# A fused attention and gated-mixer kernel on one core: groups of the mixer one place later among the heads, spatial groups half by half, and the last mixer in another order

## What is computed

```python
h = np.maximum(x @ w_in, 0.0)                       # 512 -> 1024
u, v = h[..., :512], h[..., 512:]
v_n = (v - mu) / np.sqrt(var + 1e-06)               # over the 512 columns
v_s = np.einsum('ts,bsd->btd', w_spatial, v_n) + b_spatial[None, :, None]
y = (u * v_s) @ w_out                               # 512 -> 512
```

## Time and profile before

| | us |
|---|---|
| median of 3 runs | 867.6 (867.1 to 869.02) |
| the profiled execution, its own time | 869.89 |
| its span in the trace | 868.1 |
| TensorE busy | 836.6 (96%) |
| TensorE weight loads busy | 709.4 (82%) |
| VectorE, ScalarE, GpSimd busy | 348.9 (40%), 290.5 (33%), 203.2 (23%) |

### The profile page before, as it was taken

How to read it: one execution, slowest core, us unless ns; L and a number is a source line. 1 busy time by engine, 2 the same in 40 slices (tenths; PEclk the granted TensorE clock), 3 DMA queues, 4 the chain that set the end, 5 groups by cost and what they waited for, 6 DMA issues and landing times.

```text
span 868.1 us, 13430 instructions
## 1 busy us (share of the span) xinstructions
PE 836.6 (96%) x5064; PEld 709.4 (82%) x5064; DVE 348.9 (40%) x774; ACT 290.5 (33%) x784; POOL 203.2 (23%) x289
## 2 busy tenths in 40 slices
PE   7989999999999999998989999999999999999998
PEld 4766787768877688777969999999999999999997
DVE  5876644365443664417464312213222123122111
ACT  5865654355543554424344111111111111111110
POOL 4874646243341442503341000000000000000000
PEclk9999999999999999999989999999999999999999
DMA  6551321221212221016343003003003002001000
GB/s 212 163 174 42 112 81 42 77 86 58 69 43 76 80 65 42 2 54 194 98 147 114 1 1 109 1 0 109 0 0 109 0 0 90 18 0 43 30 1 36
DMA packets 37681, 56.02 MB, mean 65 GB/s; under 512 B 2749, under 2 KB 20157, under 8 KB 37630
## 3 DMA queue, kind: packets, MB, share of 16 engines
q1 hardware_dynamic: 37630, 55.34, 19.5%
HBM read 45.90 MB, written 9.44 MB: 64 GB/s over the span
## 4 chain that ended last, share of the span: by engine, by line
PE 51%; issue 4%; POOL 1%; DVE 1%; ACT 0%; POOLq 0%; ACTq 0%; DVEq 0%
PE psum L1017 17%; PE psum L1016 17%; PE psum L1015 17%; PE psum L1083 1%; POOL rstd L494 0%; POOL unit_raw L536 0%; DVE mix_buf L820 0%; POOL x_r L503 0%; DVE units_r L864 0%; DVE y_res L921 0%; DVE units_r L866 0%; POOL probs L483 0%; DVE mix_buf L810 0%; ACT x_r L616 0%; ACT units_r L682 0%
## 5 line engine op out<-in xcount | busy, mean ns | idle before, releaser
L908 DVE SCALAR_TENSOR_TENSOR h_r<-psum,h_r 128x384 fp32r<-128x384 f32 x96 | 53.5, 557 | 287.0 <-ACT h_r L709 287.0
L709 ACT ACTIVATE h_r<-psum 128x384 fp32r<-128x384 f32 x96 | 47.2, 492 | 340.5 <-PE psum L1017 340.5
L1015 PE MATMUL psum<-xn_r,units_r 128*128 128x384 f32 x384 | 129.6, 337 | 0.0
L1017 PE MATMUL psum<-xn_r,units_r 128*128 128x384 f32 x384 | 129.3, 337 | 0.0
L1016 PE MATMUL psum<-xn_r,units_r 128*128 128x384 f32 x384 | 128.9, 336 | 0.0
L483 POOL TENSOR_SCALAR probs<-probs,row_inv 128x512 f32<-128x512 f32 (+4 forms) x160 | 95.6, 612 | 139.2 <-DVE row_inv L759 139.2
L569 ACT ACTIVATE probs<-psum,neg_max 128x512 f32<-128x512 f32 (+4 forms) x160 | 89.1, 564 | 95.9 <-DVE neg_max L746 95.7
L746 DVE TENSOR_REDUCE neg_max<-psum 128x1 f32<-128x512 f32 (+4 forms) x160 | 77.6, 535 | 92.5 <-PE psum L938 92.3
L1017 PE MATMUL psum<-units_r,h_r 128*128 128x512 f32 x288 | 113.7, 395 | 0.0
L1016 PE MATMUL psum<-units_r,h_r 128*128 128x512 f32 x288 | 113.5, 394 | 0.0
L1015 PE MATMUL psum<-units_r,h_r 128*128 128x512 f32 x288 | 111.9, 389 | 0.0
(11 more groups left out here) (101 smaller groups left out, 1477.5 us busy)
## 6 DMA issues: line engine op xcount, KB each, us to landing
qk_raw<-qk SPq DMA_DIRECT2D x32, 576.0 KB, 4.0
unit_raw<-w_ch SPq DMA_DIRECT2D x32, 256.0 KB, 3.1
y_norm<-y_scratch SPq DMA_DIRECT2D x6, 768.0 KB, 5.8
y_res<-y_scratch SPq DMA_DIRECT2D x6, 768.0 KB, 4.6
out<-y_res SPq DMA_DIRECT2D x18, 256.0 KB, 2.1
v_raw<-vN SPq DMA_DIRECT2D x16, 256.0 KB, 3.0
y_scratch<-mix_buf SPq DMA_DIRECT2D x16, 256.0 KB, 2.0
w_raw<-w_in SPq DMA_DIRECT2D x8, 256.0 KB, 4.8
```

Of the source, the lines that this page charges most:

```text
L709: act.activation(h_hi[:, f % HR, :], h_bank[:, f % 2, 0:CHUNK], ACT.Relu).then_inc(h_hi_done, 1)
L908: dve.scalar_tensor_tensor(h_lo[:, f % HR, :], h_bank[:, f % 2, 0:CHUNK], 0.0, h_hi[:, f % HR, :].bitcast(F32), ALU.max, ALU.subtract).the ...
L1015: pe.matmul(dst, a_hi, b_hi, start=start, stop=False)
L1017: return pe.matmul(dst, a_lo, b_hi, start=False, stop=stop)
```

## The change

- `groups_at` subtracts one place: each group comes one place later, the last group (w 4) of batch b at step 0 of the first head of batch b+2, and w 4 of batch 2 behind `attend(31)`, ahead of the last mixer.
- An s group i now has columns 128·(i%4) and token half i//4: all four column blocks of the first 288 tokens, then of the second. The w groups 0 and 1 (tokens 0 to 255) wait for four `gate_lo` only, w 2 for all eight. ACT now waits for all eight itself before it writes `y_stage` 0.
- Both halves of v come three steps behind their group (`split_at`), and on DVE ahead of normalisation and statistics.
- ACT empties a bank, and rounds a gate, at the head of steps 0 and 2, ahead of the exponentials; in steps 1 and 3 at the end as before, now behind the half of v.
- Last mixer: `tail_mixer` goes. For group g, ACT empties a u bank first, then rounds v of g-2, then empties other banks, then rounds the gate of g itself; DVE does the low half of v g-2, normalises v g-1, then reads g. POOL does the gate's low half at g. The transposes of y go ahead of w 3 instead of w 4. SP stores y ahead of loading a unit.
- v groups 0 and 1 each wait for their own buffer's store.

```diff
@@ groups_at, split_at
-            return [(b, sum(len(r) for r in GROUP_STEPS[:i]) + GROUP_STEPS[i].index(step))]
+            at = GROUPS * b + sum(len(r) for r in GROUP_STEPS[:i]) + GROUP_STEPS[i].index(step) - 1
+            return [(at // GROUPS, at % GROUPS)] if at >= 0 else []
...
-            return late(n, step, 2)
+            return late(n, step, 3)
@@ SyncE
+            for b, g in groups_at(HEADS, 0):
+                store_y(b, kind_of(g)[1])
             sp.wait_ge(x_lo_done, KD * B)
...
             for g in range(GROUPS):
+                if kind_of(g)[0] == "w":
+                    store_y(B - 1, kind_of(g)[1])
                 for f in unit_at(g, 2):
                     load_unit(f + US)
-                if kind_of(g)[0] == "w":
-                    store_y(B - 1, kind_of(g)[1])
@@ GpSimd, ScalarE, VectorE, TensorE: place of an s group
-                    k, d, h = NS * b + i, i // 2, slice(HALF * (i % 2), HALF * (i % 2 + 1))
+                    k, d, h = NS * b + i, i % KD, slice(HALF * (i // KD), HALF * (i // KD + 1))
@@ GpSimd, last mixer
-                tail_mixer(mixer_read, mixer_finish, g)
+                mixer_read(B - 1, g)
+                if is_kind(g, "s"):
+                    mixer_finish(B - 1, g)
@@ ScalarE, mixer_read
-                    elif b >= 1 and i == 0:
-                        for s in range(2):
-                            act.wait_ge(y_stored[s], 16 * ((k + 1 - s) // 2))
+                    elif b >= 1:
+                        act.wait_ge(y_stored[k % 2], 16 * (k // 2))
...
+                    elif i == 0:
+                        act.wait_ge(gate_lo, NS * (b + 1))
@@ ScalarE, heads
                 for step in range(STEPS):
+                    if step in (0, 2):
+                        for b, g in late(n, step, 1):
+                            mixer_read(b, g)
+                            if kind_of(g)[0] == "s":
+                                mixer_finish(b, g)
...
-                    for b, g in late(n, step, 1):
-                        mixer_read(b, g)
-                        if kind_of(g)[0] == "s":
-                            mixer_finish(b, g)
                     for b, g in split_at(n, step):
                         if kind_of(g)[0] == "v":
                             mixer_finish(b, g)
+                    if step in (1, 3):
+                        for b, g in late(n, step, 1):
+                            mixer_read(b, g)
+                            if kind_of(g)[0] == "s":
+                                mixer_finish(b, g)
@@ ScalarE, last mixer
+            for b, g in groups_at(HEADS, 0):
+                mixer_read(b, g)
...
-                tail_mixer(mixer_read, mixer_finish, g)
+                if is_kind(g, "u"):
+                    mixer_read(B - 1, g)
+                if is_kind(g - 2, "v"):
+                    mixer_finish(B - 1, g - 2)
+                if not is_kind(g, "u"):
+                    mixer_read(B - 1, g)
+                if is_kind(g, "s"):
+                    mixer_finish(B - 1, g)
                 for f in unit_at(g, 1):
...
-                if g == GROUPS - 2:
+                if g == GROUPS - 3:
                     for m in range(CT):
                         xn_tile(0, m, acc_bank)
@@ VectorE, heads
+                    for b, g in split_at(n, step):
+                        mixer_finish(b, g)
                     for b, g in late(n, step, 2):
                         normalise_v(b, g)
...
-                    for b, g in split_at(n, step):
-                        mixer_finish(b, g)
@@ VectorE, last mixer
-                tail_mixer(mixer_read, mixer_finish, g, normalise_v)
+                if is_kind(g - 2, "v"):
+                    mixer_finish(B - 1, g - 2)
+                if is_kind(g - 1, "v"):
+                    normalise_v(B - 1, g - 1)
+                mixer_read(B - 1, g)
...
-                if g == GROUPS - 2:
+                if g == GROUPS - 3:
@@ TensorE
                     if i == 0:
+                        pe.wait_ge(gate_lo, NS * b + KD)
+                    elif i == HALF // P:
                         pe.wait_ge(gate_lo, NS * (b + 1))
...
             attend(HEADS - 1)
+            for b, g in groups_at(HEADS, 0):
+                mixer(b, g)
...
-                if g == GROUPS - 1:
+                if g == GROUPS - 2:
                     transpose_xn(0, acc_bank)
                 mixer(B - 1, g)
```

More of the change, by code:

```diff
@@ L311, in bank_free, with is_kind @@
                 eng.wait_ge(copied, NCOPY * b + (g if g < S0 else g - NS) + 1)
[L313 to L323, removed]
+        def is_kind(g, kind):
+            return 0 <= g and kind_of(g)[0] == kind
         pieces = []
@@ L691, in _ @@
             for g in range(GROUPS):
-                tail_mixer(mixer_read, mixer_finish, g)
+                if is_kind(g, "u"):
[6 more added lines that the diff above has]
+                    mixer_finish(B - 1, g)
                 for f in unit_at(g, 1):
+                    if f == 0:
+                        act.wait_ge(grouped, GROUPS * (B - 1))
                     if f == AFTER_U:
@@ L1041, in mixer @@
                         pe.wait_ge(vn_lo_done, NT * (b + 1))
+                    d, h = i % KD, slice(HALF * (i // KD), HALF * (i // KD + 1))
                     c = slice(P * d, P * (d + 1))
```

## The result

| | before | after |
|---|---|---|
| median of all runs (us) | 868.3 (867.1 to 869.8) | 844.6 (843.7 to 845.4) |
| the profiled execution, its own time | 869.89 | 845.24 |
| its span | 868.1 | 843.5 |
| first scores of head 9 / `attend(31)` | 59.58 / 385.96 | 59.05 / 366.81 |
| first matmul of layer 3 | 457.10 | 432.42 |

The ratio is 0.9725 with a 95% interval from 0.9704 to 0.9747. The forecast was 844.5.

The account below looks back on a forecast made before the run. It took the kernel as TensorE-bound with fourteen holes: 17.8 us of holes, 2.1 of start-ups and 7.5 of clock, 27.4, less 4.3 of new losses, net 23.1, giving 844.5 us from 867.6; range 840 to 853.

Parts of the forecast that it names:

- All fourteen holes close: TensorE's named waits in heads and last mixer all go: 11.0 + 6.8 = 17.8 us, plus 2.1 of start-ups.
- Clock in the heads, 3.2 us: Behind two of three holes at the first w group the clock was low; closing them gives 3.2 us.
- Two new holes at u 1 and u 4: Last mixer: TensorE waits 0.65 us at u 1 and 1.5 at u 4, released by ACT.
- the walk: Last mixer followed from w 4's start with set times per operation: waits sum to 2.3 us, 2.7 with start-ups.
- the first rival: Last mixer keeps its hole: POOL's units lengthen five normalisations, u 1 and u 4 wait 6 us; 849 us, chance 0.20.
- Clock: Last mixer: half of the 1.5 us of clock, 0.8 us, allowed as lost behind the new holes.
- the halves do nothing in the heads: Heads: the shift alone separates s 7 from w 0, so the time is the same and only the credit moves.
- v's halves later: Heads: halves a step later, so two waits for exponentials, 1.1 us, go, with 0.5 us left over for the unseen.
- Emptying ahead of exponentials: Heads: ACT's bank read of 0.4 to 0.6 us fits ahead at no cost and closes three u holes, 0.8 us.
- Transposes 0.3 lost, SP's order free: Last mixer: transposes ahead of w 3 wait 0.3 us; SP's stores ahead of loads free `y_stage` earlier, some units load later.
- Slower: Heads: ACT stands at steps 0 behind a bank or store, exponentials come late, over 0.97 us per head; 870.5, chance 0.04.
- a wait in the heads: Rival: the wait moves inside the heads, TensorE waits 0.3 us in each of 24, 7 us; 851.5 us, chance 0.16.

Follow-up runs that it names:

- the kernel with later units: The changed kernel with units 0, 1 and 2 scaled behind groups 5, 7 and 9 instead of 1, 3 and 5; 843.3 us.
- the run with the old last order: The changed kernel with the last mixer's earlier order of work on ACT, DVE and POOL; 846.1 us.
- the run with SP's old order: The changed kernel with y's transposes ahead of w 4 again and SP loading a unit ahead of storing y; 848.0 us.
- without the halves: The changed kernel with s groups in the old order of columns and token halves, w 0 waiting for all eight gates; 853.2 us.
- The place alone: The kernel before with one edit, every group one place later; 875.7 us, ratio 1.0062.
- the halves alone: The kernel before with s groups half by half, w 0 and w 1 waiting for four gates and w 2 for eight; 857.7 us.
- v later on top of the shift: The kernel before with groups one place later and, in the heads, v's halves three steps behind and ahead of normalisation and statistics on DVE; 866.8 us.

## Why the prediction was right, and where its reasons were wrong

In the total it was right, and so it was stretch by stretch: it gave 15.35 us to the heads (11.0 of holes, 1.65 of start-ups, 3.2 of clock, less 0.5), where 15.8 were found, and 7.75 to the last mixer (6.8, 0.45, 4.3 of clock, less 2.7, 0.8, 0.3), where 8.4 were. That it lies within 0.1 us of the median is luck: single terms, below, miss by more than 1 us, one way and the other.

- *All fourteen holes close, PE waits for no gate and no x in the heads.* Right; nothing at all is left in the heads, where 0.5 was allowed.
- *Clock in the heads, 3.2 us.* Behind the holes at w 0 it came back: from 67 us to `attend(31)` the granted clock is 0.99 before and 1.00 after. But from 59 to 67 us it is 0.79 before and 0.59 after, 1.6 us lost where nothing was reckoned with, so about 1.6 are left of the term. The heads gained 15.8 all the same: with the 0.5 that was not needed, about 1.5 us stand in no term of the sum, and where they lie is open.
- *Two new holes at u 1 and u 4, 0.65 and 1.5 us.* The places are right, both released by ACT; they measured 1.71 and 1.70. The mis-sized term is u 1's: the walk took 0.68 us for each subtraction, and one took 1.53. At u 4 the size is near by luck: the walk had 1.5 without any lengthening, and had the 2.40 us subtraction taken 0.68, everything from it to ACT's emptying would have come 1.7 us earlier and next to nothing of that hole would be left (an estimate from the rows above). This is the mechanism of the first rival at about a third of its price: it had 6 us of waits, the forecast 2.15, and 3.4 came. It had the five normalisations lengthened, and it was the subtraction, by 0.85 and 1.72 us. The rule of the Trainium skill that the prediction weighed (GPSIMD Engine Reference, Key points) names contention of POOL with DVE's instructions of two SBUF inputs, as the subtraction is; the trace agrees, with 4.33 us beside four units in the kernel with later units.
- *Clock.* 0.8 us was taken off for a low clock behind the new holes; it stayed at 1.00. The hole of 2.60 us in before and the one of 2.59 in the run with the old last order had a lower clock behind them, holes of 1.7 here did not. The length alone does not decide it: behind the 2.6 us hole ahead of layer 3 in the run with SP's old order the clock was 1.00 (435 to 445 us). The clock that stayed up made up for what the holes had grown.
- *The shift alone closes the w 0 hole, "even without the next part", and the halves do nothing in the heads.* Wrong. The shift alone makes the kernel slower by 5.9 us of span (1.4 of them clock around 60 us), and without the halves 4.3 us of the wait come back. The step looked at PE's list only: it counted the scores and transposes that cover the chain, and not the same head's work on ACT and POOL, which comes into the chain.
- *v's halves later close 1.1 us in the heads.* As a part of the change this is wrong: 5.6 us in the heads from one end and about 7 from the other. The hole they close does not stand in the earlier trace rows, because it is the shift that opens it.
- *Emptying ahead of exponentials: 0.8 us.* About 2.5 were found, of which 0.9 is in named waits; the cover holds, since no head pays for it.
- *Transposes 0.3 lost, SP's order free.* The first is 0. The second is the wrong one: SP's order was taken to matter for units only. Together with the halves the old order holds the y store behind a load and costs 2.6 us; this hole was not in before because the 3.5 us hole at w 0 stood in front of it and gave the store time. The traces bear this out without a run for it alone: in before the second y store is issued 3.3 us behind the first (445.27, 448.61) and ACT waits for no store; with the halves alone it is 7.0 us (429.63, 436.65) and ACT stands 4.6.
- *Slower* and *a wait in the heads* didn't come about in the whole change. The place alone shows how near it was: three waits of up to 3 us. (The 870.5 that the prediction had for *slower* is 844.5 and 24 times 1.1, which makes 870.9.)

The parts do not add: shift +5.9, halves −12.4, v later on top of the shift −8.5, all from spans. That the sum was right while two of its credits were wrong is because the sum asked which holes stay at the end, and all parts together close them; it would have misjudged any half of the change.

Left open: why the same code at 60 us gets either level of clock; the 1.5 us of the heads that no term has; the 1.0 us that emptying late costs beside named waits; and whether the shift is worth anything in the changed kernel. The last was not tried, since the kernel that differs from the changed one by it alone was not run. The wait for x that it closes is 3.4 us in the kernel with the halves alone, which is the nearest number.

## What to carry to other kernels

When work is moved between two dependent steps to cover a latency, follow the moved work through every engine's list: what covers on TensorE may stand in the chain on GpSimd or ScalarE, and a 2.3 us chain became 6.0. Value a part of a schedule from both ends, alone and missing from the whole, because a part that loses alone may be one that another part needs. Where an idle engine has optional work, hold it back from the critical stretch: here one wait on GpSimd, with three units listed six groups later, took away both remaining holes and 4 us. Listing them four groups later without the wait did not.

## What the runs showed of the hardware

- A subtraction of two 128x512 float32 operands on VectorE took 0.69 us alone, 1.53 beside one GpSimd multiplication of the same size, 2.40 beside two and 4.33 beside four, which took 4.03 themselves. GpSimd kept its pace of 1.0 to 1.1 us in these, and VectorE all but stood until it had ended. In each of these the GpSimd operation, or the first of them, had started ahead of the subtraction. Where VectorE was under way first, GpSimd paid too: the unit below took 1.48 us beside a subtraction that had started 0.71 us ahead of it (and was itself held by a gate's subtraction on GpSimd until 411.54).

```profile
410.79 1.30 DVE L879 TENSOR_TENSOR units_r<-unit_raw,units_r 128x512 fp32r<-128x512 f32 x1
411.50 1.48 POOL L529 TENSOR_TENSOR unit_raw<-unit_raw,g_cols 128x512 f32<-128x512 f32 x1
```

- The granted clock from 60 to 65 us was 0.50, 0.61 to 0.66 or 1.00 in kernels whose code is the same up to there, worth up to 3 us of 840.
- A store queued behind a load whose buffer is not free waits with it: it was issued at 428.96, 7.4 us behind the store before it, where in the other order both were issued within 2.9 us.
